# Moving one of seven matmul groups and the order of the weight splits in the last stage of an attention and experts kernel

## What is computed

```python
# 1. decaying linear attention per head
state = gamma * state + k[t] outer v[t];  y[t] = scale * q[t] @ state
# 2. one expert of 8 per token
out[mask] = gate_w[mask, None] * (np.maximum(x[mask] @ w1[e], 0.0) @ w2[e])
# 3. a bilinear layer
a = x @ w1
b = x @ w2
h = a * b @ w3
return (h @ w_out).astype(np.float32)
```

## Time and profile before

| | us |
|---|---|
| median of three runs (lowest, highest) | 850.59 (849.52, 853.0) |
| the profiled execution, one of these three | 853.0 |
| its span, first to last instruction | 851.1 |
| TensorE busy | 823.1 (97%) |
| VectorE busy | 414.7 (49%) |
| ScalarE busy | 292.4 (34%) |
| GpSimd busy | 176.5 (21%) |

### The profile page before, as it was taken

The page is one execution under the profiler, slowest core; times in us unless marked ns, Lnnn a source line. Parts: engine busy times, 40 slices in busy tenths (PEclk is TensorE's granted clock), DMA queues, the critical chain, the costliest instruction groups (busy, mean ns, idle before and its releaser), DMA issues.

```text
span 851.1 us, 14864 instructions
## 1 busy us (share of the span) xinstructions
PE 823.1 (97%) x5578; PEld 705.3 (83%) x5579; DVE 414.7 (49%) x662; ACT 292.4 (34%) x467; POOL 176.5 (21%) x207
## 2 busy tenths in 40 slices
PE   9899999998999999999998899999999999999995
PEld 8899878787999998888886678888888888888884
DVE  3667788630213144111142887762577742778400
ACT  1234423331222244212143545522545423454210
POOL 2223002202020120201001334311433311433011
PEclk9999999999999999999999899999999999999999
DMA  9999992423030343210231211141112231111010
GB/s 324 326 316 314 290 352 94 149 100 101 0 100 0 99 148 116 81 49 20 79 114 59 62 52 50 50 149 50 51 51 73 81 106 49 63 50 50 12 50 37
DMA packets 51456, 91.88 MB, mean 108 GB/s; under 512 B 8529, under 2 KB 15313, under 8 KB 51409
## 3 DMA queue, kind: packets, MB, share of 16 engines
q1 hardware_dynamic: 41728, 68.47, 24.0%
q0 software_dynamic: 4736, 14.72, 5.2%
q10 hardware_dynamic: 4946, 8.08, 2.8%
HBM read 71.03 MB, written 20.22 MB: 107 GB/s over the span
## 4 chain that ended last, share of the span: by engine, by line
PE 89%; DVE 6%; issue 2%; ACT 1%; ACTq 1%; DVEq 0%; POOL 0%
PE bank L444 35%; PE attn L444 32%; PE pair L444 8%; PE bank L970 3%; PE attn L997 3%; PE pair L982 3%; PE pair L1075 2%; PE bank L1009 1%; PE attn L988 1%; PE bank L947 1%; PE bank L1158 1%; ACTq L393 1%; DVE wlo L1255 0%; DVE w3T L1255 0%; PE pair L954 0%
## 5 line engine op out<-in xcount | busy, mean ns | idle before, releaser
L444 PE MATMUL bank<-xT,we_p 128*128 128x512 f32 (+1 forms) x672 | 141.9, 372 | 4.9 <-issue 3.6
L444 PEld LDWEIGHTS bank<-xT,we_p 128*128 128x128 f32 x672 | 124.5, 192 | 21.9 <-issue 6.0
L444 PE MATMUL attn<-hT,we_p 128*128 128x512 f32 (+1 forms) x672 | 141.8, 368 | 0.0
L444 PEld LDWEIGHTS attn<-hT,we_p 128*128 128x128 f32 x672 | 121.3, 188 | 14.4
L444 PE MATMUL attn<-wc,gT 128*128 128x512 f32 x576 | 132.5, 390 | 0.2
L444 PEld LDWEIGHTS attn<-wc,gT 128*128 128x128 f32 x576 | 107.9, 188 | 23.8 <-DVE gT L1255 1.5
L1501 DVE SCALAR_TENSOR_TENSOR hT<-bank,hT 128x512 fp32r<-128x512 f32 x56 | 38.7, 691 | 152.7 <-ACT hT L741 152.7
L444 PE MATMUL bank<-yhi,whi 128*128 128x512 f32 x240 | 94.6, 394 | 3.4 <-issue 3.4
L444 PE MATMUL bank<-yhi,wlo 128*128 128x512 f32 x240 | 94.1, 392 | 0.0
L741 ACT ACTIVATE hT<-bank 128x512 fp32r<-128x512 f32 x56 | 33.5, 599 | 104.3 <-PE bank L444 104.3
L635 POOL TENSOR_TENSOR w_raw<-a,w_raw 128x256 f32<-128x256 f32 x24 | 23.9, 994 | 184.1 <-DMA w_raw<-in_moe_w_dram 184.1
(11 more groups left out here) (198 smaller groups left out, 1218.6 us busy)
## 6 DMA issues: line engine op xcount, KB each, us to landing
we_raw<-in_moe_w_dram SPq DMA_DIRECT2D x6, 2048.0 KB, 9.4
w_raw<-in_moe_w_dram SPq DMA_DIRECT2D x40, 256.0 KB, 2.7
yT_sorted<-yout ACTq DMA_DIRECT2D x7, 1024.0 KB, 4.8
qkv<-in_q_t_dram SPq DMA_DIRECT2D x24, 256.0 KB, 3.4
qkv<-in_v_dram SPq DMA_DIRECT2D x24, 256.0 KB, 5.1
x_rows<-x_keep SPq DMA_DIRECT2D x24, 256.0 KB, 3.5
qkv<-in_k_t_dram SPq DMA_DIRECT2D x23, 256.0 KB, 5.0
qkv<-in_k_dram SPq DMA_DIRECT2D x20, 256.0 KB, 5.2
```

The lines of the kernel that those rows point to most:

```text
L444: i = pe.matmul(out_, left(a), right(b), start=(first and n == 0), stop=(last and n == 2), **kw)
```

## The change

Four things are edited.

- On TensorE, `third(n)` of the last quad of a phase is called right after that quad, not between the fourth and fifth block of the first output rows.
- On ScalarE, each quad's three w_hi parts for the next quad stand one place earlier: part 0 before p_one, part 1 before g_hi of group 0, part 2 before u_two.
- On ScalarE, w_hi(1, 0) moves from the end of the last window to the head of the first quad, behind the loop.
- On VectorE, w_lo(1, 0) moves from the end of the last window's block to quad 0, behind c11(0) and y_lo(0, 6).

```diff
--- before.py
+++ after.py
@@ -815,7 +815,6 @@
                     y_store(w, start, BANK)
                     with act.If(total < w + 2):
                         p_one_copy(0)
-                        w_hi(1, 0)
 
                 def one_tile_hidden():
                     this = is_new(act, w)
@@ -892,6 +890,7 @@
                 copy(otile[:, n % 2, :], bank[4 + n % 2][:, :], scale=meta_in[:, n:n + 1, 1:2].rearrange("p a b -> p (a b)")).then_inc(s_o, 1)
 
             def first_quad():
+                w_hi(1, 0)
                 u_two_copy(0)
                 y_hi(0, 6)
                 w_hi(1, 1)
@@ -901,16 +900,16 @@
 
             def quad(n):
                 more, behind = n + 1 < NQ, n % KF > 0
+                if more:
+                    w_hi(n + 1, 0)
                 p_one_copy(n)
                 if more:
-                    w_hi(n + 1, 0)
+                    w_hi(n + 1, 1)
                 if behind:
                     g_hi(n - 1, 0)
                 if more:
-                    w_hi(n + 1, 1)
+                    w_hi(n + 1, 2)
                 u_two_copy(n)
-                if more:
-                    w_hi(n + 1, 2)
                 if behind:
                     g_hi(n - 1, 1)
                 u_three_copy(n)
@@ -1211,8 +1210,6 @@
                 if n >= 2:
                     pe.wait_ge(s_o, n - 1)
                 for f in range(KF):
-                    if j + t == 0 and f == GT:
-                        third(p * KF + KF - 1)
                     if t == 0:
                         pe.wait_ge(s_glo, 2 * (p * KF + f) + j + 1)
                     i = product(pe, bank[4 + n % 2][:, :], lambda a: gT[j][:, a, f, t * P:(t + 1) * P], lambda a: wc[:, a, f, :],
@@ -1222,6 +1219,7 @@
             for p in range(NP):
                 for n in range(p * KF, (p + 1) * KF):
                     quad(n)
+                third(n)
                 for n in range(p * TP, (p + 1) * TP):
                     out_rows_of(n)
 
@@ -1545,7 +1543,6 @@
                 y_lo(0, 4)
                 y_lo(0, 5)
                 w_lo(0, 2)
-                w_lo(1, 0)
 
             def window(w, total):
                 def wide_hidden():
@@ -1630,8 +1627,7 @@
                 if n == 0:
                     y_lo(0, 6)
                 if more:
-                    if n:
-                        w_lo(n + 1, 0)
+                    w_lo(n + 1, 0)
                     w_lo(n + 1, 1)
                 if behind:
                     g_lo(n - 1, 0)
```

## The result

| | median us | lowest to highest | runs |
|---|---|---|---|
| before | 850.06 | 848.66 to 853.0 | 4 |
| changed | 856.88 | 856.77 to 857.12 | 4 |

The ratio of changed to before is 1.0077, with a 95% interval of 1.0047 to 1.0107: 6.8 us slower, against 7.6 predicted. The table has four executions of each; the record lists thirteen of the changed kernel, between 854.3 and 861.2. The profiled execution of the changed kernel took 857.9, its span is 855.9.

The account below looks back on a forecast made before the run. TensorE, busy 97% of the span, was taken as the bound. Terms 4.0 + 2.1 + 1.0 + 0.5 = 7.6 us on the median 850.6 gave 858.2, range 854.2 to 862.5.

Parts of the forecast that it names:

- Part 1: End of each eight quads: moved factor 3 waits for c22, losing 1.74 less 0.40 recovered from g_lo; 4.0 us for three.
- Part 2: Steady quads: p_one behind w_hi part 0 delays factor 6 by w - 0.42, w being the DMA wait; 2.1 us.
- Part 3: First quad of the second and third eight: p_one, already late, goes behind part 0; 0.52 lost twice, 1.0 us.
- Part 4: Quads 0 and 1: later w_lo(1, 0) costs 2.30 ahead of factor 1, covering factor 3's old 1.80 stall; net 0.5 us.
- Rival B: TensorE's clock falls to 0.50 behind a new stall; one fall gives 860.2, one at each of four 866; chance 0.07.
- A: ScalarE's copy order is free because loads land earlier; steady-quad and later first-quad losses vanish; 855.1; chance 0.12.
- C: Loads land later in the new kernel's executions, by 0.2 in every quad; 861; chance 0.12.
- D: Not slower: at the ends of the eights TensorE does not reach factor 3 before c22; 849.9; chance 0.03.
- three signs of being wrong: Wrong if last-stage TensorE stalls total under 4 us, clock leaves 1.00 after 482, or u_two or g_lo releases a matmul.

Follow-up runs that it names:

- factor 3 alone: Kernel before with only factor 3 of each phase's last quad moved to directly behind that quad; ratio 1.0042.
- ScalarE's order alone: Kernel before with only ScalarE's new order of w_hi parts inside quads 1 to 23, first quad as before; ratio 1.0007.
- changed, first: First trace of the changed kernel, its profiled execution, nothing else altered; 857.9 us.
- factor 3 put back: Changed kernel with factor 3 returned to its place among the output matmuls, both other edits kept; ratio 1.0025 to the kernel before.
- changed, again: Changed kernel run again unaltered for a second trace; 858.96 us, ratio 1.0096 to the kernel before.
- w_lo alone: Kernel before with only w_hi(1, 0) and w_lo(1, 0) moved behind the loop; ratio 1.0014.
- before, again: Kernel before run again unchanged for a second trace; ratio 0.9994.
- four repeats: Kernel before with only w_hi(1, 0) and w_lo(1, 0) moved behind the loop, plus four repeats of c11(0) ahead of the real one; 855.3 us, one run.

## Why the prediction was right, point by point

| term | predicted | trace of the changed kernel | edit alone |
|---|---|---|---|
| 1. factor 3, three times | 4.0 | 5.3 - 1.1 = 4.2 | 3.9 |
| 2. steady quads | 2.1 (1.4 to 3.5, least 0) | 1.0; 3.4 in the second trace | 0.7 |
| 3. first quads of later phases | 1.0 | 1.0 | 1.0 |
| 4. quads 0 and 1 | 0.5 (to 1.25) | 2.1; 0.4 in the second trace, without the fall | 0.7 |
| sum, in the stage | 7.6 | 8.3; 9.0 in the second trace | |

The third column is against the first trace of before, the last against the mean of its two.

**Part 1** held almost to the hundredth: 1.74 from one chain of rows and the rule taken from a stall elsewhere, against 1.74 to 1.77. In the rows above, the weight load starts with its matmul, at 556.85, behind c22's end at 556.79, and the second step is 0.33 as in the earlier trace rows. The Trainium skill (TensorE: Matmul & The Clock Gate, section "Architectural detail: the array is 16× 32×32, not 1× 128×128") says that TensorE's queue can pull weight loads ahead of matmuls in flight. No load was pulled ahead of this wait, which it shares with its matmul. The 0.40 was recovered as said; at the two other ends it was 0.36 to 0.38.

**Part 2** had the right mechanism and threshold; what failed is taking one trace's waits as the size. The trace of before that I read has an excess of 2.07, a second of the same kernel 0.00. The 19 waits in it are not 19 independent samples of what the next trace does: their whole level moves between traces (mean 0.49 and 0.30 for before, 0.29 and 0.52 for the changed kernel), and by chip or set more than within one, as the table of excesses shows. The range down to 0 covered what came. Why the level moves was not tried. u_two and g_lo cost nothing in the steady quads, as said.

**Part 3** was exact. I had it that a later u_two would hide inside the same shift; with part 0 left behind p_one it shows by itself and costs the same 0.51.

**Part 4** is the step that failed. "w_lo(1, 0) takes the slot after y_lo, from 488.71 to 489.66" holds as a time after quad 0's start: 12.57 was said, 12.5 measured, so the way out of the loop does get earlier. But I left TensorE's arrival where the one trace had it, and it moves with the low clock at quad 0's start. Slow stretch and stall must be taken together: 4.49 with the edit, against 4.06 (first trace of before) and 3.5 to 3.55 (its second, factor 3 alone, ScalarE's order alone) without it. So the net is 0.4 to 1.0, about 1.0 in most. The first trace was the odd one by 0.54, see the last section.

**Rival B** came true once: I gave it 0.07. It came in two of the four traces that have both the moved w_lo(1, 0) and nothing in front of it added (changed, first; factor 3 put back) and in neither of the others (changed, again; w_lo alone). In both, quad 0's slow stretch had been of the short kind (1.5), which makes the stall of the long kind. So the edit does not only cost 1.0, it opens a stall that now and then also costs 1.6. Whether the length decides is not shown: behind 2.74 and 2.76 idle the clock fell, behind 2.70 it did not, three lengths too close to tell, and the 2.70 came after a long slow stretch (2.98), so the two are not told apart. What separates them stays open. The 1.5 idle stalls of part 1 never brought a fall, in four traces with three each.

**A, C and D**: A has two halves. Loads early enough to make part 2 free stand in one trace (before, again: excess 0.00), but part 3 cost its 1.0 in every trace with part 0 ahead. C's late loads came in the second trace. D's precondition, a chain shorter than the last matmul's tail, appeared nowhere.

**The sum against the median.** In the stage the traces say 8.3 and 9.0; the runs say 6.8 (4.0 to 9.1 by the interval from 1.0047 to 1.0107) and 8.2. They agree within scatter. The three edits alone add up to 6.0 in the stage; most of the changed kernel's remainder is the clock's 1.6 in its first trace and the late loads (2.7) in its second. That the first trace's 8.3 lies so near 7.6 is partly luck: part 2 came 1.1 under its term, and part 4 came 1.6 over, by a fall of the clock that the sum did not hold.

**The signs.** Of the three signs of being wrong, one came: the clock left 1.00 after 482 in the first trace (0.69 in 486:488), though not in the second. TensorE's stalls were over 4 us, and neither u_two nor g_lo released a matmul. In the steady quads p_one starts 1.6 later on average in the first trace (1.7 was said), the waits for the loads are 1.65 each (1.85 was said), and one steady quad, not nine, shows idle time released by p_one; the other losses are in the steps alone.

## What to carry to other kernels

Where an engine runs dense, cost a reordering by slack at each moved instruction: when its feed ends, when the next matmul is due, and a fixed amount for restarting. A copy that empties an accumulator should not stand behind an instruction that waits for a DMA, even if it has waited there "for nothing" so far. And before a term is sized from waits near a threshold, read them in a second trace of the same kernel, if possible on another chip: their level was not the kernel's.

## What the runs showed of the hardware

- A matmul that restarts after a wait costs more than the wait: its second matmul starts 0.39 after the feed's end, where 0.227 is the spacing. In the changed kernel it was 0.39 behind c22 (556.10 + 0.69, then 557.18) and 0.40 behind p_one (549.00 + 0.58, then 549.98).
- A short VectorE subtraction of 128x256, w_lo(1, 2), took 0.95 where it ran into GpSimd's sums (from 490.02 on) in the first trace of before, and 0.42 in the second, where it ended 0.2 after they began. That is the 0.54 by which c22(0) was later there. The two rows, first trace of before and second (`x2` merges w_lo(1, 1) and w_lo(1, 2)):

```profile
489.46 1.82 DVE L1255 TENSOR_TENSOR wlo<-w_raw,whi 128x768 fp32r<-128x768 f32 x2
```

```profile
483.83 1.28 DVE L1255 TENSOR_TENSOR wlo<-w_raw,whi 128x768 fp32r<-128x768 f32 x2
```

The Trainium skill (GPSIMD Engine Reference, section "1. Specifications") says that GpSimd's SBUF interfaces are shared with VectorE and contend with VectorE instructions that have two SBUF inputs, as this subtraction has. The rows agree, 0.95 against 0.42, and so does the trace with four repeats, y_lo 1.70 against 1.22.
- Behind stalls of nearly one length the granted clock differed: 1.00 behind 2.70 idle, 0.50 soon after 2.74 and 2.76.
